# Attention of an attention-and-experts kernel: six tiles of a batch for heads 0 to 3, then for heads 4 to 7

## The reference

```
k_sum = k.reshape(B, H, nb, block, D).max(axis=3)      # block = 32, nb = 24
v_sum = v.reshape(B, H, nb, block, D).mean(axis=3)
scores_l = scale * q @ k^T, kept where |i - j| < 16
scores_s = scale * q @ k_sum^T + log(32)
a = softmax(concat(scores_l, scores_s))
x = a @ concat(v, v_sum)                               # 1536 rows of 8 * 64 = 512
```

## Time and profile before

| | |
|---|---|
| median of 3 runs | 569.95 us (568.17 to 576.67) |
| the profiled execution | 572.47 us, of which span 570.7 us |
| mean granted TensorE clock | 0.958 |
| attention and gate logits | 0 to 103.0 us |
| routing | 103.0 to about 117 us |
| experts and dense layers | about 117 to 570.7 us |

### The profile page before, as it was taken

How to read it: one execution, slowest core, us unless ns; L and a number is a source line. 1 busy time by engine, 2 the same in 40 slices (tenths; PEclk the granted TensorE clock), 3 DMA queues, 4 the chain that set the end, 5 groups by cost and what they waited for, 6 DMA issues and landing times.

```text
span 570.7 us, 9187 instructions
## 1 busy us (share of the span) xinstructions
PE 529.0 (93%) x3152; PEld 433.3 (76%) x3153; DVE 281.6 (49%) x535; ACT 255.3 (45%) x539; POOL 71.9 (13%) x108
## 2 busy tenths in 40 slices
PE   4799998169999999899979999999999999999997
PEld 3377777158888889788867888888888888888885
DVE  3568775635523444754205723754642663642631
ACT  4468776224433434653304633631643550553520
POOL 6314510232014013120200000000000000000000
PEclk9979999568999999989998999999999999999999
DMA  9999641259047046561352063053164041330001
GB/s 211 225 207 227 162 117 51 62 195 350 25 162 239 19 174 216 197 221 36 148 176 83 3 218 148 1 185 121 63 221 147 0 165 61 142 147 0 0 18 55
DMA packets 75386, 74.16 MB, mean 130 GB/s; under 512 B 45408, under 2 KB 47456, under 8 KB 75360
## 3 DMA queue, kind: packets, MB, share of 16 engines
q1 hardware_dynamic: 71072, 62.28, 36.4%
q0 software_dynamic: 2560, 8.39, 4.6%
q10 hardware_dynamic: 1728, 3.15, 1.6%
HBM read 63.32 MB, written 10.49 MB: 129 GB/s over the span
## 4 chain that ended last, share of the span: by engine, by line
PE 84%; SPq 4%; ACT 3%; DMA 3%; issue 3%; DVE 2%; POOL 1%; POOLq 0%; ACTq 0%; DVEq 0%
PE psum L1173 13%; PE psum L1174 12%; PE psum L1175 12%; PE psum L1189 12%; PE psum L1187 12%; PE psum L1188 12%; PE psum L1055 2%; PE psum L1088 2%; ACT p_sb L594 2%; PE psum L1071 2%; PE psum L1142 1%; PE psum L1046 1%; SPq L309 1%; PE psum L1030 1%; DMA k_nat<-in_k 1%
## 5 line engine op out<-in xcount | busy, mean ns | idle before, releaser
L1173 PE MATMUL psum<-xT_hi,w_hi 128*128 128x512 f32 (+1 forms) x320 | 124.0, 388 | 4.1 <-DVE w_lo L902 2.3
L1174 PE MATMUL psum<-xT_lo,w_hi 128*128 128x512 f32 (+1 forms) x320 | 123.5, 386 | 0.0
L1175 PE MATMUL psum<-xT_hi,w_lo 128*128 128x512 f32 (+1 forms) x320 | 123.1, 385 | 0.0
L1187 PE MATMUL psum<-w_hi,h_hi 128*128 128x512 f32 x296 | 115.9, 392 | 0.0
L1189 PE MATMUL psum<-w_hi,h_lo 128*128 128x512 f32 x296 | 115.2, 389 | 0.0
L1188 PE MATMUL psum<-w_lo,h_hi 128*128 128x512 f32 x296 | 115.2, 389 | 0.0
L902 DVE TENSOR_TENSOR w_lo<-w_raw,w_hi 128x512 fp32r<-128x512 f32 x80 | 51.4, 686 | 60.7 <-ACT w_hi L651 60.5
L1173 PEld LDWEIGHTS psum<-xT_hi,w_hi 128*128 128x128 f32 x320 | 61.6, 193 | 16.8 <-DVE xT_lo L912 5.0
L1175 PEld LDWEIGHTS psum<-xT_hi,w_lo 128*128 128x128 f32 x320 | 61.6, 193 | 11.9
L1174 PEld LDWEIGHTS psum<-xT_lo,w_hi 128*128 128x128 f32 x320 | 61.7, 193 | 11.6
L671 ACT ACTIVATE h_small<-psum 128x512 f32<-128x512 f32 x48 | 28.7, 598 | 89.9 <-PE psum L1175 89.9
(11 more groups left out here) (134 smaller groups left out, 530.7 us busy)
## 6 DMA issues: line engine op xcount, KB each, us to landing
w_raw<-in_moe_w_in SPq DMA_DIRECT2D x12, 1024.0 KB
w_raw<-in_moe_w_out SPq DMA_DIRECT2D x6, 2048.0 KB, 8.3
w_raw<-in_moe_w SPq DMA_DIRECT2D x8, 1024.0 KB
w_raw<-in_moe_w SPq DMA_DIRECT2D x4, 2048.0 KB, 8.9
vw<-in_v SPq DMA_DIRECT2D x20, 192.0 KB, 4.9
k_nat<-in_k SPq DMA_DIRECT2D x12, 256.0 KB, 5.1
q_nat<-in_q SPq DMA_DIRECT2D x12, 256.0 KB, 5.1
x_rows<-x_cur ACTq DMA_DIRECT2D x12, 256.0 KB, 3.8
```

The lines of the kernel that those rows point to most:

```text
L1173: mm(h, w1_hi[:, c, cols], xT_hi[:, c, 0:n], start=(c == 0), stop=False)
L1174: mm(h, w1_hi[:, c, cols], xT_lo[:, c, 0:n], start=False, stop=False)
L1175: last = mm(h, w1_lo[:, c, cols], xT_hi[:, c, 0:n], start=False, stop=(c == KD - 1))
L1187: mm(y_ps[s % 2], h_hi[:, c, rows], w2_hi[:, c, :], start=(c == 0), stop=False)
```

## The change

A batch now takes its six tiles for heads 0 to 3 (units 0 to 5), then for heads 4 to 7 (units 6 to 11); batch 1 likewise in units 12 to 23. So the prologue needs only four of the eight pieces of k and half of the mean of v. The other pieces are worked in the loop, at the units that `K_UNIT` lists (two of them in unit 3), the other halves of the mean at the units of `MEAN_UNIT`. The transposed q of six tiles stays in `q_cur`, and x of six tiles in `x_cur`, until the second group of heads is through. A tile's x is whole only in the second pass over the tiles, so `transpose_x`, `gate_logits` and the stores of x fall in units 7 to 12 and 19 to 23, one of each in every unit. `gate_logits` stands now directly ahead of the products of `weighted_v`, and writes to the bank of its result. `transpose_q` for tiles 3 to 5 is in units 0 to 2, for tiles 6 to 11 in units 9 to 14. Loads of k, strips and v are cut in two by heads, so there are twice as many DMAs with half the size; their packets stay 256 bytes (1536 instead of 768 for batch 0's v). GpSimd makes batch 0's zeros in k and the mask before the ones and zeros of v.

```
+GROUP_PIECES = PIECES // 2
+K_UNIT = {4: 1, 5: 2, 6: 3, 7: 3, 8: 6, 9: 7, 10: 8, 11: 9, 12: 12, 13: 13, 14: 14, 15: 15}
+Q_AHEAD = 3
+Q_UNIT = {t: t - Q_AHEAD if t < QT else B_UNITS + t - QT - Q_AHEAD for t in range(Q_AHEAD, T)}
+MEAN_UNIT = {4: (0, 1), 10: (1, 0), 16: (1, 1)}
+def unit(n):
+    b, rest = divmod(n, B_UNITS)
+    g, i = divmod(rest, QT)
+    return b, g, i, b * QT + i
+def last_unit(t):
+    b, i = divmod(t, QT)
+    return b * B_UNITS + QT + i
...
-        q_cur = att("q_cur", [P, 2, PAIRS, P])
+        q_cur = att("q_cur", [P, QT, PAIRS, P])
...
-        lg_ps = psum[:, 5, 0:E]
+        lg_ps = [psum[:, 4, 264:264 + E]] * (T - 2) + [psum[:, i, 0:E] for i in (3, 6)]
-        kt_banks = [7, 5, 6, 4]
-        kt_ps = [psum[:, kt_banks[m % 4] if m < PIECES else 3, 0:KHALF] for m in range(B * PIECES)]
+        kt_banks = [7, 6, 4, 2] + [5] * GROUP_PIECES + [3] * PIECES
+        kt_ps = [psum[:, bank, 0:KHALF] for bank in kt_banks]
...
+            load_k(0, 0, 0)
+            load_k(0, 0, 1)
+            load_q(0)
+            load_q(1)
+            load_v(0)
+            sp.wait_ge(zeros_ready, 5)
+            load_strips(0)
+            load_q(2)
+            load_k(0, 1, 0)
+            load_strips(1)
+            load_q(3)
+            load_k(0, 1, 1)
+            load_strips(2)
+            load_q(4)
+            load_v(1)
+            load_strips(3)
+            load_q(5)
             sp.dma_start(w_gate[:], moe_w_gate.rearrange("(c p) e -> p c e", p=P)).then_inc(gate_loaded, 16)
+            load_strips(4)
+            load_strips(5)
+            load_strips(6)
+            load_k(1, 0, 0)
+            load_strips(7)
+            load_k(1, 0, 1)
...
             def transpose_k(m):
                 b, half, pr = piece(m)
-                pe.wait_ge(k_loaded[b][half], 16 * KJ)
+                pe.wait_ge(k_loaded[b][pr // (HG // 2)][half], 16 * KJ)
+                if m == GROUP_PIECES:
+                    pe.wait_ge(vsum_ready, 1)
+                elif m > GROUP_PIECES:
+                    pe.wait_ge(ksum_maxed, m)
...
             def weighted_v(n):
+                b, g, i, t = unit(n)
                 pe.wait_ge(pt_ready, n + 1)
+                pe.wait_ge(v_loaded[n], 32)
+                pe.wait_ge(vsum_ready, n + 1)
                 if n >= 1:
                     pe.wait_ge(x_ready, n)
+                for t_ in range(T - 2):
+                    if last_unit(t_) + 2 == n:
+                        gate_logits(t_)
...
-            for m in range(PIECES):
+            for m in range(GROUP_PIECES):
                 transpose_k(m)
-            pe.wait_ge(zeros_ready, 9)
             transpose_q(0)
+            scores(0)
             transpose_q(1)
-            scores(0)
             scores(1)
-            mean_first()
+            mean_first(0)
+            transpose_q(2)
             for n in range(UNITS):
                 transpose_p(n)
-                if K_STEP <= n < V_STEP:
-                    transpose_k(PIECES + n - K_STEP)
+                if n in MEAN_UNIT:
+                    b, g = MEAN_UNIT[n]
+                    if b:
+                        mean_second(g, n)
+                    else:
+                        mean_first(g)
+                for m in K_UNIT:
+                    if K_UNIT[m] == n:
+                        transpose_k(m)
                 if n + 2 < UNITS:
                     scores(n + 2)
-                if g == 0 and t >= 1:
-                    transpose_x(t - 1)
-                if g == 1 and t >= 1:
-                    gate_logits(t - 1)
-                if g == 1 and t + 2 < T:
-                    transpose_q(t + 2)
-                if n == V_STEP + 1:
-                    mean_second()
+                for t in range(T - 1):
+                    if last_unit(t) + 1 == n:
+                        transpose_x(t)
+                for t in Q_UNIT:
+                    if Q_UNIT[t] == n:
+                        transpose_q(t)
                 weighted_v(n)
+            gate_logits(T - 2)
             transpose_x(T - 1)
             gate_logits(T - 1)
```

More of the change, by code:

```diff
@@ L284, in piece @@
         def piece(m):
-            return m // PIECES, m % PIECES // PAIRS, m % PAIRS
+            b, rest = divmod(m, PIECES)
+            g, rest = divmod(rest, GROUP_PIECES)
+            half, pr = divmod(rest, HG // 2)
+            return b, half, g * (HG // 2) + pr
         block = ctx.enter_context(nc.Block())
@@ L302, in load_strips, with load_k @@
                     part = NSUM + lo - (s * STRIP - WINDOW)
-                    sp.dma_start(vw[part:part + hi - lo, b, s, :, 0:D],
-                                 v[b, :, lo:hi, :].rearrange("h p d -> p h d")).then_inc(v_loaded[t], 16)
-            def load_k(b, half):
+                    sp.dma_start(vw[part:part + hi - lo, b, s, heads, 0:D],
+                                 v[b, heads, lo:hi, :].rearrange("h p d -> p h d")).then_inc(v_loaded[n], 16)
+            def load_k(b, g, half):
+                heads = slice(g * HG, (g + 1) * HG)
@@ L307, in load_k @@
                 for j in range(KJ):
                     rows = slice((half * KJ + j) * P, (half * KJ + j + 1) * P)
[L309 to L315, removed]
@@ L331, in _ @@
[L331 to L342, removed]
+                    sp.dma_start(k_nat[:, b, half, j, heads],
+                                 k[b, heads, rows, :].rearrange("h p d -> p h d")).then_inc(k_loaded[b][g][half], 16)
@@ new lines, in _ @@
+            load_strips(5)
[3 more added lines that the diff above has]
+            load_k(1, 0, 1)
+            sp.wait_ge(zeros_ready, 9)
+            for n in range(8, UNITS):
+                sp.wait_ge(x_ready, n - 6)
+                if n == 8:
+                    load_v_rows(0)
+                if 9 <= n < 15:
+                    load_q(QT + n - 9)
+                load_strips(n)
+                if n in (12, 14):
+                    load_k(1, 1, (n - 12) // 2)
+                if n == 15:
+                    load_v_rows(1)
@@ L424, in fill, with fill_v, fill_k @@
                 pool.wait_ge(zeros_ready, filled[0])
-            fill(vw[:, :, :, :, D:D + 1], 1.0)
-            for b in range(B):
+            def fill_v(b):
                 fill(vw[0:64, b, 0, :, 0:D], 0.0)
                 fill(vw[96:128, b, STRIPS - 1, :, 0:D], 0.0)
-            for b in range(B):
+            def fill_k(b):
                 fill(kw[:, :, b, 0, NSUM:NSUM + WINDOW], 0.0)
                 fill(kw[:, :, b, STRIPS - 1, COLS - WINDOW:], 0.0)
[L436 to L445, removed]
+            fill_k(0)
             chain(nc.gpsimd.memset(mask[:, :, :, 0:NSUM], -math.log(BLOCK)))
```

262 lines of the change are left out of this document (141 added, 121 removed).

## The result

The changed kernel has a median of 580.94 us (579.91 to 581.11, 4 runs); the kernel before has 569.06 (566.60 to 576.67, 4 runs). The ratio is 1.022, with a 95% interval of 1.018 to 1.026: slower by 12 us, where 3.5 were forecast and 579.5 was the top of the range. The profiled execution is 581.09 us, 8.6 more than that of before, which lay above its own median. Some executions run slower, at a lower granted clock: the ratios are of the fast ones alone, the medians of all. The last logits come at 111.93 us instead of 102.85; what follows them takes 467.4 us instead of 467.8. So in this pair of executions all of it is in attention, 9.1 us there against 3.5 in the forecast. In which stage the median executions differ by the other 3 us isn't shown.

The account below looks back on a forecast made before the run. PE, busy 529.0 of 570.7 us, was taken as the bound, with only attention's end movable. Last values 3.2 us later, tail 0.6 gained, clock 0.9 lost: 3.5 later, median 569.95 becoming 573.5; range 566 to 579.5.

Parts of the forecast that it names:

- The start's gain: Prologue: less k and half the mean, so first transposed probabilities at 16.2 instead of 21.51; surviving-gain rival 0.25, 565.5 to 570.
- What the loads leave of it: Units 1 and 2: with bytes and packets as price, q of tile 5 lands at 26.1, unit 3 begins at 27.3.
- A rule that spoke against the step: Loads: the skill advises larger DMAs; estimated 0.8 of the rate at 128 KB, landing 6 us later, time about 580.
- The price by DMA: Rival, loads: each DMA costs 1.06 us whatever its size, q of tile 5 lands at 35.7, time 583; chance 0.08.
- The loop: Unit 3 to the last values: unit times sum to 74.1 us, ending at 101.4 instead of 98.2, 3.2 later.
- The clock: Units 1 to 4: waits may halve the clock and slow unit 4's mean; 0 to 4 us, 0.9 taken.
- feared it in units 16 to 19: Rival, units 16 to 19: the clock falls where PE has 1.8 of 2.48 us; 4.2 us more, 577.7; chance 0.12.
- The tail: Last values to last logits: gate_logits(10) fills PE's wait for the last normalisation, gaining 0 to 1.5 us, 0.6 taken.

Follow-up runs that it names:

- the first experiment: Changed kernel with q of tile 5 loaded ahead of the second half of batch 0's v and unit 3's strips: 577.94 us, ratio 1.015 to the kernel before.
- the one on the pieces: Changed kernel with batch 0's pieces 4 to 7 of k worked one each in units 0 to 3: 576.22 us, ratio 1.013 to the kernel before.
- the one on the logits: Changed kernel with the gate logits ahead of q's transposes again: 577.37 us, ratio 1.014 to the kernel before.
- the two that removed the wait for q of 3.28 us: Changed kernel with q of tile 5 loaded earlier, 577.94 us; changed kernel with batch 0's v loaded in packets of 768 bytes, 578.99 us.
- the kernel before with the busy prologue: Kernel before plus 22 unread 128x128 products on TensorE ahead of its first transpose_k: 571.42 us, ratio 1.006 to the kernel before.
- the three edits together: Changed kernel with q of tile 5 loaded earlier, pieces one each in units 0 to 3, logits ahead of q's transposes: 572.15 us, ratio 1.005 to kernel before.

## Why the prediction was wrong

The direction was right and the size was not. The forecast had the last logits at 102.85 + 3.5 = 106.35 us; they came at 111.93, 5.6 later. Two terms of its sum failed, both ahead of unit 3: the landing of q of tile 5, and the gain of the start. By its own steps:

- **The start's gain** (5.3 us, first probabilities at 16.2): measured 1.6, at 19.92. The first scores were at 11.36 instead of 10.3, the half mean began at 14.36 instead of 12.9, and it took 5.14 us where 2.7 was halved from a row at full clock. By PE alone unit 3 could then begin at 28.8 (the estimate under the first experiment) and not at 24.9. So even with the load at 26.1 unit 3 would have been 1.5 us behind the forecast's 27.3, where the forecast had the load decide.
- **What the loads leave of it** is the step that failed: "If bytes and packets are the price, q of tile 5 lands at 26.1", and unit 3 begins at 27.3. It landed at 30.48 and unit 3 began at 32.59. That is the 1.5 us of the start and 3.8 of the load: a wait of 3.3, and 0.9 because q's transposes and the values then ran at half clock, less 0.4 that PE would have waited for ACT otherwise. The load wasn't issued late (21.41); it took 9.03 us instead of 5.07, the last 4.4 of them at 106 GB/s. The landing varies by 2.4 us among kernels with the same loads, and 30.48 is the latest of them; all five are about 2 us or more behind the 26.1 of the forecast. Why is open. Halved DMAs made another load late by 2.5 us in one execution of the kernel before and by 1.1 in one with all its loads cut, but there by being issued late, so their share here isn't shown. The load of v in packets of 1536 bytes may be a part: cut into 768 it was followed by a landing at 27.3, in one execution. The order of the loads wasn't tested apart from the cuts.
- **A rule that spoke against the step** was weighed and not followed. The Trainium skill (DMA: Bandwidth & Descriptors, the measured bandwidths) has smaller DMAs slower, in a table for DMAs issued from GpSimd; from it the forecast estimated a factor of 0.8, a landing 6 us later and 580 us. The traces agree in direction: in the kernel before with halved loads the rate from 22 to 28 us fell from 214 to 182 GB/s, a factor of 0.85, and in the changed kernel that of the first 26.08 us from 219 to 206, 0.94. That its 580 us is near the measured 580.94 is in part luck, since some 2 of the 5.6 us come from other terms.
- **The price by DMA** in its strong form (1.06 us for each) is refuted: SP had q of tile 5 issued by 21.9 us, 28 DMAs in 21.1 us with 1.6 us of waiting for the fills among them. The kernel before needed as long for its nineteen: the last of them goes out from 21.01 to 22.17 us, where the forecast took the end of the eighteenth, 20.97, for it. (Counted out, q of tile 5 is itself the last of the 28.)
- **The loop** was right in its sum, in part by errors that cancel: 74.1 us from unit 3 to the last values were forecast, with 0.9 for the clock 75.0, and 75.8 were measured. Against the same units at full clock in other kernels here, the clock cost 2.4 of them (units 3, 4, 13 and 14), so at full clock the loop is 73.4. Single units up to 22 were within 0.4 us where the clock was full (unit 8: 3.48 against 3.70; 9: 4.64 against 4.83; 11: 3.59 against 3.92; 16 to 19: 2.65, 2.47, 2.48, 2.47 against 2.48).
- **The clock** was the right mechanism, undersized and misplaced. It was half from about 29.3 to 39.3 us (the stretches above and the rows at 30.48 to 38.74), and for some 3 us in units 13 and 14; the forecast feared it in units 16 to 19, where PE does less and where it stayed full. Of the edits, the one on the pieces and the one on the logits gave more by their medians than the 2.0 and 2.1 us that they took out of the units at full clock; the two that removed the wait for q of 3.28 us gave less.
- **The tail** gained 1.05 us where 0.6 was taken. It is the clock and not the moved logits: where the clock was full to the end, the tail took 3.5 us in both orders, in the kernel before with the busy prologue and in the three edits together.

The sum: 5.3 late at unit 3, 0.8 in the loop, 0.45 back in the tail, 5.65. The medians are 12 us apart rather than 8.6, because the profiled execution of before was one of its slower ones.

So the change bought a shorter prologue, which in the profiled kernel before was hidden behind the wait for a load, and paid with loads on which its first units wait, with steps on the circle of the loop, and with idle time that lets the clock fall. With the pieces spread, the logits moved, the prologue kept busy, and banks and half mean arranged anew, the same order of units costs nothing and gains nothing.

## What to carry to other kernels

Ask of a shortened prologue which load the first waiting unit needs, and count that load's place in the queue; that the bytes ahead are the same doesn't fix its landing, which here came 4.4 us later behind the same bytes. Where engines execute in order, place steps so that each wait for a shared bank has other work ahead of it and no unit has two of the same kind: a wait of 1.5 us costs its length, and here it was more than once followed by a fall of the clock, which the next long step pays. Price a moved step at both levels of the clock if idle time stands ahead of it.

## What was not expected of the hardware

- The same load at the same place in the queue took 6.9 to 9.0 us from issue to landing in five kernels whose loads don't differ; in the slowest the DMA rate was 30 GB/s for a microsecond, with the load still open. A landing that decides is worth more than one look.
- DMAs of 128 and 96 KB in place of 256 and 192, with the same packets, moved 182 to 194 GB/s in place of 208 to 214, in one execution. The issue of one took SP 0.5 us or more; 96 KB in 0.5 us is 197 GB/s, so it may be SP's issuing that held the rate there (an estimate; no run separates it).
- A wait of 1.69 us and one of 0.60 in the unit ahead, with PE busy for 3.95 of 6 us, were followed by a half mean of 5.05 us in place of 2.7: all of it ran at 1.2 GHz.
- What follows the last logits, untouched, took 462.7 us in one execution, 464.6 and 465.2 in three, and 467.1 to 468.0 in the other ten: a spread larger than what most edits here were worth.
